# Attention in whole tiles: both groups' scores together, their turnings and weighings around them

## What is computed

```python
scores = q @ k.T / sqrt(64) + bias            # bias = -slope_h * distance, masked outside the window
a = exp(scores - max); a = a / (sum(a) + 1e-9)
x = a @ v                                     # (B, S, 512)
h = x.T @ U @ V                               # rank 32, over the positions
u = x + h.T
x = u + relu(u @ w_ch1) @ w_ch2               # 512 -> 2048 -> 512
hdn = relu(x @ w_in); uu, vv = split(hdn)
vv = w_spatial @ normalise(vv) + b_spatial
out = (uu * vv) @ w_out
```

## Time and profile before

| | us |
|---|---|
| median of 3 executions | 530.94 (528.90 to 530.97) |
| profiled execution | 530.2 |
| its span | 528.4 |
| TensorE busy in the span | 515.6 (98%) |
| VectorE, ScalarE, GpSimd busy | 191.3, 181.7, 125.4 |
| mean granted TensorE clock | 0.983 of full |

### The profile page before, as it was taken

The page is one execution under the profiler, slowest core; times in us unless marked ns, Lnnn a source line. Parts: engine busy times, 40 slices in busy tenths (PEclk is TensorE's granted clock), DMA queues, the critical chain, the costliest instruction groups (busy, mean ns, idle before and its releaser), DMA issues.

```text
span 528.4 us, 7432 instructions
## 1 busy us (share of the span) xinstructions
PE 515.6 (98%) x2808; PEld 440.7 (83%) x2808; DVE 191.3 (36%) x538; ACT 181.7 (34%) x446; POOL 125.4 (24%) x120
## 2 busy tenths in 40 slices
PE   4999999999999999999999999999999999999997
PEld 4799979888788888888888888888888998888996
DVE  6566667722123423121111312112375355440440
ACT  4677788742323321021101233222443212332121
POOL 6477678334333500000000043323000000000000
PEclk8599999999999999999999999999999999999999
DMA  8540641003223210000000022230000000110002
GB/s 241 179 137 2 198 163 42 2 5 117 81 87 111 81 40 1 0 1 1 1 0 1 0 81 89 60 120 19 1 1 2 0 1 0 61 40 21 1 20 99
DMA packets 12245, 27.85 MB, mean 53 GB/s; under 512 B 2225, under 2 KB 2225, under 8 KB 12209
## 3 DMA queue, kind: packets, MB, share of 16 engines
q1 hardware_dynamic: 10480, 24.22, 14.2%
q10 hardware_dynamic: 1728, 3.15, 1.6%
HBM read 24.22 MB, written 3.15 MB: 52 GB/s over the span
## 4 chain that ended last, share of the span: by engine, by line
PE 94%; POOL 2%; DVE 1%; issue 1%; DMA 1%; ACT 0%; DVEq 0%; POOLq 0%; ACTq 0%
PE bank L988 28%; PE bank L1175 25%; PE bank L1163 25%; PE bank L1038 7%; PE bank L1008 4%; PE bank L1021 3%; PE bank L1045 1%; POOL w_slot L421 1%; DVE bias L495 1%; PE bank L1070 1%; PE bank L1059 1%; DMA cfg_i<-in_cfg 1%; POOL qk_split L382 0%; ACT prob L787 0%; DVE qk_split L492 0%
## 5 line engine op out<-in xcount | busy, mean ns | idle before, releaser
L1175 PE MATMUL bank<-hid,w_slot 128*128 128x512 f32 x576 | 139.2, 390 | 0.0
L1163 PE MATMUL bank<-u_split,w_slot 128*128 128x512 f32 x576 | 138.4, 389 | 0.0
L1175 PEld LDWEIGHTS bank<-hid,w_slot 128*128 128x128 f32 x576 | 107.7, 188 | 23.2 <-issue 0.9
L1163 PEld LDWEIGHTS bank<-u_split,w_slot 128*128 128x128 f32 x576 | 107.7, 188 | 22.4
L659 DVE SCALAR_TENSOR_TENSOR hid<-bank,hid 128x512 fp32r<-128x512 f32 x48 | 33.2, 691 | 192.3 <-ACT hid L885 192.3
L885 ACT ACTIVATE hid<-bank 128x512 fp32r<-128x512 f32 x48 | 28.7, 598 | 203.4 <-PE bank L1163 203.4
L787 ACT ACTIVATE prob<-prob,row_min 128x256 f32<-128x256 f32 (+1 forms) x96 | 45.8, 479 | 18.4 <-DVE row_min L510 18.4
L421 POOL TENSOR_TENSOR w_slot<-stage,w_slot 128x1024 fp32r<-128x1024 f32 x16 | 38.2, 2388 | 52.3 <-ACT w_slot L841 52.3
L988 PE MATMUL bank<-sp_slot,vn 128*128 128x384 f32 x288 | 50.3, 334 | 0.0
L988 PEld LDWEIGHTS bank<-sp_slot,vn 128*128 128x128 f32 x288 | 50.0, 188 | 0.2
L1038 PEld LDWEIGHTS bank<-v_all,probT 128*128 128x128 f32 x352 | 43.2, 198 | 2.6 <-issue 1.8
(11 more groups left out here) (89 smaller groups left out, 455.7 us busy)
## 6 DMA issues: line engine op xcount, KB each, us to landing
stage<-in_w_ch SPq DMA_DIRECT2D x16, 512.0 KB, 3.3
qk_raw<-in_qk SPq DMA_DIRECT2D x24, 256.0 KB, 4.5
v_all<-in_v SPq DMA_DIRECT2D x12, 256.0 KB, 5.1
out_dram<-o_stage ACTq DMA_DIRECT2D x12, 256.0 KB, 2.0
stage<-in_w_spT SPq DMA_DIRECT2D x6, 384.0 KB, 3.0
stage<-in_w_in SPq DMA_DIRECT2D x4, 512.0 KB, 3.3
stage<-in_w_out SPq DMA_DIRECT2D x2, 512.0 KB, 3.5
V_raw<-in_V SPq DMA_DIRECT2D x4, 96.0 KB, 4.1
```

Of the source, the lines that this page charges most:

```text
L1163: last = mm(h_bank[g % 2][:], w_slot[f][:, a, k * P:(k + 1) * P], u_split[c][:, m, k, :], start=(k == 0 and p == 0), stop=(k == KD - 1 and ...
L1175: last = mm(c_ring[(KD * c + k) % 6][:], w_slot[f][:, a, 512 + k * P:512 + (k + 1) * P], hid[g % 2][:, m, :], start=(f == 0 and a == HI an ...
```

## The change

Each engine's loop now takes a tile instead of a group. On TensorE: turn(2t), [gather_z at t = 7, mix(t-8) from t = 8], scores(2t+2), scores(2t+3), [fold_z at t = 7], turn(2t+1), weigh(2t), turn_x(t-1), weigh(2t+1). On VectorE take_x(2t) is the last of tile t and take_x(2t-1) the first of the next. On ScalarE `split_stage` comes at the end of tiles 4, 5, 6, `round_u` at the end of tiles 8 to 11. On GpSimd `split_u` comes two groups later and the last behind the loop. No instruction is added, removed or changed in shape.

```diff
@@ gpsimd
-                    if g >= 17 and g % 2:
-                        split_u((g - 17) // 2)
+                    if g >= 19 and g % 2:
+                        split_u((g - 19) // 2)
+                split_u(KD - 1)
@@ vector
-                for s in range(-2, QUADS + 1):
-                    if 0 <= s - 1 < QUADS:
-                        take_x(s - 1)
-                    if 0 <= s < QUADS:
-                        take_probT(s)
-                        invert(s)
-                    if s in (15, 17, 19, 21):
-                        sum_u((s - 15) // 2)
-                    if 0 <= s + 2 < QUADS:
-                        score_bias(s + 2)
-                    if s == 13:
+                for t in range(-1, TILES + 1):
+                    now, ahead = 0 <= t < TILES, t + 1 < TILES
+                    if t >= 1:
+                        take_x(2 * t - 1)
+                    if now:
+                        take_probT(2 * t)
+                        invert(2 * t)
+                    if 8 <= t < TILES:
+                        sum_u(t - 8)
+                    if ahead:
+                        score_bias(2 * t + 2)
+                    if now:
+                        take_probT(2 * t + 1)
+                        invert(2 * t + 1)
+                    if ahead:
+                        score_bias(2 * t + 3)
+                    if t == 7:
                         split_z(0)
+                    if now:
+                        take_x(2 * t)
@@ scalar
+                for t in range(-1, TILES):
+                    now, ahead = t >= 0, t + 1 < TILES
+                    if now:
+                        add_eps(2 * t + 1)
+                        take_probT(2 * t)
+                    if t == 7:
                         copy_z(0)
+                    if ahead:
+                        exps(2 * t + 2)
+                    if t == 7:
                         round_z(0)
+                    if now:
+                        take_probT(2 * t + 1)
+                    if ahead:
+                        add_eps(2 * t + 2)
+                        exps(2 * t + 3)
+                    if t >= 1:
+                        take_xT(t - 1)
+                    if 4 <= t < 7:
+                        split_stage(t - 4)
+                    if 8 <= t:
+                        round_u(t - 8)
@@ tensor
+                for t in range(-1, TILES):
+                    now, ahead = t >= 0, t + 1 < TILES
+                    if now:
+                        turn(2 * t)
+                    if t == 7:
                         pe.wait_ge(x_half, 2 * NT)
                         pe.wait_ge(xT_sb, NT)
                         pe.wait_ge(U_in, 16)
                         gather_z(0)
+                    if t >= 8:
+                        pe.wait_ge(V_split, 2)
+                        pe.wait_ge(xT_sb, t - 1)
+                        mix(t - 8)
+                    if ahead:
+                        scores(2 * t + 2)
+                        scores(2 * t + 3)
+                    if t == 7:
                         pe.wait_ge(fold_set, 1)
                         fold_z(0)
+                    if now:
+                        turn(2 * t + 1)
+                        weigh(2 * t)
+                    if t >= 1:
+                        pe.wait_ge(x_half, 2 * t)
+                        if t == 7:
                             pe.wait_ge(z_split, 1)
+                        elif t > 7:
+                            pe.wait_ge(u_sum, t - 7)
+                        elif t > 1:
+                            pe.wait_ge(xT_sb, t - 1)
+                        turn_x(t - 1)
+                    if now:
+                        weigh(2 * t + 1)
```

More of the change, by code:

```diff
@@ L1091, in _ @@
             with pe.If(near):
-                for s in range(-2, QUADS):
-                    if s >= 0:
-                        turn(s)
-                    if s == 13:
+                for t in range(-1, TILES):
[3 more added lines that the diff above has]
+                    if t == 7:
                         pe.wait_ge(x_half, 2 * NT)
```

33 lines of the change are left out of this document (removed).

## The result

| | before | changed |
|---|---|---|
| median of 8 executions each | 530.96 | 533.46 |
| lowest to highest | 528.9 to 532.04 | 532.38 to 536.11 |
| profiled execution (span) | 530.2 (528.4) | 534.16 (532.3) |
| TensorE at hidden(0) | 110.66 | 114.63 |

The changed kernel is 2.5 us slower: ratio 1.0057, 95% interval 1.0035 to 1.008.

A forecast was written before the change was run, and what follows sets the result against it. TensorE was taken as the bound, with 94% of the chain of waits. Terms 1.8 + 0.3 + 1.2 + 3.2 - 0.3 = +6.2, taken as +6.0, gave 536.3 us profiled, 536.9 as a median; range 533.7 to 540.0.

The forecast's parts named there:

- Tile 3: In tile 3, scores(9) wait for GpSimd's copy of k, behind its split of V: +1.2 us.
- Tiles 6 and 7: Waits of 1.18 in tile 6, 2.3 (fold_z, third stage) and 1.0 (turn_x) in tile 7, less old waits and switches: +3.2.
- The even weighing's wait: weigh(2t+1) waits for VectorE's take_x(2t): 0.84 us after the even weighing, 0.43 covered by turn_x, a wait of 0.41.
- Tail: From the last tile's turning to hidden(0): 6.65 us where it had been 6.95, so -0.3.
- the price of the second scores: On TensorE, the second of two scores in a row costs 0.91 us like the first; lower bound 0.68.
- the usual tile: Tiles 1 to 5 and 8 to 10: +0.41 wait, -0.19 switches, net +0.22 us each, +1.8 in eight.
- rival B: The second scores run as parallel pairs: 0.23 us less in eleven tiles, 2.5 in all, 534.4; chance 0.12.
- tile 0 and the clock: Tile 0, at half clock without turn_x: 0.84 less the switch, part coming back as the clock rises at the same time: +0.3.
- rival A: TensorE's clock rises early: full by 16 us, 533.6; late form, at 18.5 us, gain 2.6, 534.3; chance 0.15.
- C: Rival: tile 7 isn't held by the third weight stage, 2.0 us less: 534.9; chance 0.07.
- E: Rival: VectorE or a queue held to be in time is late, 0.1 to 0.3 us in ten tiles, up to 539; chance 0.10.
- D: Rival: the clock falls in tile 7 while TensorE idles, +5 us: 541.9; chance 0.08.

The follow-up runs named there:

- e2: The changed kernel with GpSimd's second split of V at g = 7 instead of 6; 534.18 us, ratio 1.0059.
- e1: The changed kernel with ScalarE's third weight stage at the end of tile 7 instead of 6, GpSimd's half two groups later; 531.87 us, ratio 1.0027.
- e12: The changed kernel with the edits of e1 and e2, and VectorE's take_x(12) ahead of score_bias(15); 530.67 us, ratio 0.9988.
- e5: The changed kernel with turn(2t+1) between the two scores of a tile; 536.66 us, ratio 1.0107.
- e4: The kernel before, with tile 0 alone in the new order on TensorE, VectorE and ScalarE; 529.48 us, ratio 0.9981.
- e11: e1 with tile 0 in the old order on TensorE, VectorE and ScalarE; 533.03 us, ratio 1.0035.
- e13: The changed kernel again, unaltered; 535.73 us, ratio 1.007, its profiled execution 541.62 us.
- e3: The changed kernel with weigh(2t) ahead of turn(2t+1) on TensorE and take_x(2t) ahead of take_probT(2t+1) on VectorE; 537.16 us, ratio 1.0106.
- e6: The changed kernel with tile 0 alone in the old order on TensorE, VectorE and ScalarE; 534.3 us, ratio 1.0086.
- e10: e4 with ScalarE's second weight stage one step later, behind exps(15) instead of exps(14); 536.42 us, ratio 1.0109.
- e8: The changed kernel with e1, e2, take_x(12) before score_bias(15), split_z and take_x(14) before score_bias(17), round_z before exps(16); 531.71 us, ratio 1.0032.
- e14: e12 with ScalarE's copy take_xT(5) ahead of the epsilon add of scores(14) and the exps of group 15; 529.32 us, ratio 0.9974.

## Why the prediction was right in sign and too high

**Right.** The terms that I had worked out as queues on one engine came out within 0.2:

- Tile 3: +1.2 in the sum; +1.37 in the trace, a wait of 1.07 for copy_k behind split_V. e2 removed it.
- Tiles 6 and 7: +3.2, with waits of 1.18, 2.3 and 1.0; +3.05, with waits of 1.09, 2.21 and 0.86. e1 removed the second, and e12 the first. (The sum had put the 0.2 for k_glob here, which falls into tile 8, and the 0.2 for a mixing that tile 7 loses into the tail; the two cancel.)
- Tile 8: -0.22 for GpSimd's copy. The tile took 0.25 less, where tiles 9 and 10 took 0.06 and 0.04 more, so the copy was worth about 0.3.
- The even weighing's wait: 0.84 from its end to the next weighing; 0.79. Tail: hidden(0) 6.65 behind the turning; 6.69, which is less only by 0.06 than before instead of 0.3, since 0.2 of that term was the mixing that tile 7 loses.
- Nothing changed behind hidden(0).

**The first step that failed: the price of the second scores.** "So I price the second scores like the first, 0.91, the lower bound being 6 x 0.113 = 0.68." They take 0.71 (1.62 - 0.91). I had taken 0.152 a pair from a row in which every scores stands between two switches, so that the switch out was in the price, and then kept it where there is no switch. That is 0.2 in each tile in which TensorE is the bound: the usual tile cost +0.04 to +0.09 where I had +0.22, and tiles 2 to 10 with all their waits cost +4.44 where I had 5.94. It was rival B, to which I gave 0.12, and whose bound from the earlier trace rows was the nearer row: a product that streams without a switch. e5 shows the saving as 0.20 in the scores, apart from the switches on either side. The Trainium skill (TensorEngine Tiling (Array Packing), Key Properties) says that different tiles of the array load and multiply in parallel; this trace agrees: the second six pairs take 0.71 us, 0.118 a pair, where one product of this width streams in some 0.113.

**The second: tile 0 and the clock.** "Part of it comes back, as the clock rises at the same time: +0.3." It rose 6.4 us behind the first turning instead of 11.6, and tiles 0 and 1 took 16.14 where they had taken 18.06: -1.92 against my +0.5. This is the late form of rival A, "the gain is 2.6". My argument against it was that dense work from 15 to 25 us had not lifted the clock; it told only of the old order. e4 and e11 against e1 show that the order of tile 0 moves the mean clock in most executions; why it does is not shown, and rival A's reason, denser work, isn't either: the clock was back early in e5 too, where the scores stand apart.

The forecast of 536.3 for the profiled execution is a slip of 0.1 (530.2 + 6.0 = 536.2), and the terms add up to 6.16. Together: tiles 0 and 1 were 2.44 too high, tiles 2 to 10 1.50 too high, the tail 0.24 too low; 3.70 in all, and 6.16 - 3.70 is the +2.46 of the profile. The medians have +2.5. Both rivals came in one kernel, and for that the prediction had no number: priced as they were, A's late form and B together take 5.1 off and give 531.8, within 0.5% of before. It stayed slower because B is worth less than I had priced, 0.2 only in the tiles in which TensorE is the bound and not 0.23 in eleven. So the sign was no luck of the waits, which came as forecast, but its margin was thinner than the 0.83 that I gave to "slower by over 0.5%".

The two parts can be held apart by the clock. Where both kernels had a mean granted clock of 0.987, the changed one took 533.9 to 534.2 us (4 executions) and the one before 528.3 to 529.7 (11). The new order by itself thus costs about 5 us, near what I forecast; but the kernel before is rarely at 0.987 and mostly at 0.980 to 0.984, where it takes 529.8 to 533.1, the middle one 531.0. At 0.990 the distance is the same: 532.4 to 533.0 in six of seven executions against 527.0 to 528.2 in three. The earlier clock gives about half of the 5 back.

**Of the rivals.** C and E did not happen: the stage held tile 7 in full, and no engine was late in every tile. D did not in the first profile and did in another (e13); the profiles of e2, e3, e5 and e6, with waits of 1.9 to 2.6 us where it fell or just ahead of it, have it too, and that of e10 with its wait of 4.62, while those of e1, e8, e12 and e14, where fold_z doesn't wait, have not. It isn't certain with such a wait either: the first profile had 2.21 and no fall. I had given it 0.08 on the ground that a wait of 0.92 hadn't lowered the clock; for the wait of 2.3 that I forecast this was too thin a ground. One sign of being wrong did come: tile 5, without mixing, took 7.73, under 7.8, but the scores that it computes are those of the half-sized tile 6, and it had taken 7.64 before.

## What to carry to other kernels

Price a run of equal work from a row that streams without a switch, not from a piece whose ends are both switches. When an order is made denser, go through every queue of the other engines for an instruction that is there for its own data (a staged weight, a copy for a later step): what had been free at its old place holds all that stands behind it. A new order that loses may be a good order with four such instructions in the wrong place; taking out one wait shows the next, so expect two or three rounds before the gain is seen.

## What the runs showed of the hardware that I had not expected

- The stretch at half clock at the start varies between kernels, and between executions of one kernel: it was 13.7 us long in the changed kernel's first profile and 10.2 in its second (e13), 10.2 in those of e1, e2, e4, e5, e8, e10, e12 and e14, 13.7 in e6, 17.1 before and in e3, 20.5 in e11, all with TensorE at work nearly without a pause in the later part of it.
- In the middle of dense work the clock can fall again in a wait of a few microseconds or shortly behind it, and it then stays at 1.2 GHz for 3.4 us (e2) to 17.1 us (e13), nearly all of it with TensorE busy. The price can be several times the wait: 7.6 us for a wait of 3.15 in e13. In the first tiles it fell again for 3.4 us, 0.8 to 1.2 us behind waits of 1.13 (e13) and 1.23 (e4, e14) for take_x(0), and not behind those of 0.59 to 0.98; tile 1 then took 9.30 to 9.37 instead of 7.85. But waits of 1.25 and 1.26 in tile 7 (e8, e12) and the one of 2.21 did not lower it, so the length of the wait doesn't settle it.
- VectorE's answer to a finished product came 0.27 us after its last slot, and TensorE's start 0.10 to 0.14 after VectorE's end (53.78 to 54.05, 54.47 to 54.57, and the earlier trace rows); a dependence that goes over and back costs about 0.4 beside the work itself.
- Where several semaphores are waited for, the bracket can name an engine that ended at about the same time (GpSimd's v for take_x), or none ("issue" for ScalarE's xT_sb). For the first, the program settled it: which copy the weighing needs, and that this one had long been done. For the second, e14 moved the suspected copy, and the wait went.
